# A routed-expert kernel: the first expert's weight pieces in another order, one of them split before the gathers, small copies moved on VectorE

## What is computed

```python
# 1. gated linear attention with B,H,S,D = 4,8,768,40, step by step over t; its result is x
x = attn_out.transpose(0, 2, 1, 3).reshape(B * S, H * D)      # 3072 tokens x 320
# 2. experts: N=3072 tokens, E=8 experts, F=1024, cap = N // E = 384
order = np.argsort(-(x @ w_gate).flatten())
for idx in order:
    tok, e = idx // E, idx % E
    if assigned[tok] >= 0 or counts[e] >= cap: continue
    assigned[tok] = e; counts[e] += 1
for e in range(E):
    mask = assigned == e
    out[mask] = np.maximum(x[mask] @ w1[e], 0.0) @ w2[e]
# 3. a second layer pair on all tokens, width 2048
h = out @ w_in
result = np.where(h > 0, h, np.exp(np.minimum(h, 0)) - 1) @ w_out
```

## Time and profile before

| what | us |
|---|---|
| median of three runs | 873.57 |
| lowest, highest | 872.84, 879.42 |
| the profiled execution, its own time | 876.62 |
| its span, first to last instruction | 874.3 |
| TensorE matmul busy | 806.4 |
| VectorE, ScalarE, GpSimd busy | 547.0, 461.0, 403.1 |
| mean granted clock of TensorE, share of full speed | 0.977 |

### The profile page before, as it was taken

How to read it: one execution, slowest core, us unless ns; L and a number is a source line. 1 busy time by engine, 2 the same in 40 slices (tenths; PEclk the granted TensorE clock), 3 DMA queues, 4 the chain that set the end, 5 groups by cost and what they waited for, 6 DMA issues and landing times.

```text
span 874.3 us, 17610 instructions
## 1 busy us (share of the span) xinstructions
PE 806.4 (92%) x5979; PEld 746.0 (85%) x5979; DVE 547.0 (63%) x1446; ACT 461.0 (53%) x981; POOL 403.1 (46%) x468
## 2 busy tenths in 40 slices
PE   1999999998977999999999999999999999999994
PEld 1888888887766888989998998998999899999894
DVE  7476868685754766676586577658657765543441
ACT  1544444431231576278457737836762882784573
POOL 6544444552352166246526526543651663475133
PEclk9999999998976999999999999999999999999998
DMA  3766666632331122212112121211112212021000
GB/s 61 152 136 138 137 136 131 136 80 76 103 97 30 43 65 63 65 44 58 55 47 71 46 65 46 67 62 42 59 46 65 61 52 77 28 76 50 1 1 22
DMA packets 138506, 60.94 MB, mean 70 GB/s; under 512 B 104704, under 2 KB 136704, under 8 KB 138432
## 3 DMA queue, kind: packets, MB, share of 16 engines
q1 hardware_dynamic: 136128, 52.13, 24.7%
q0 software_dynamic: 2304, 7.87, 2.8%
HBM read 51.72 MB, written 8.26 MB: 69 GB/s over the span
## 4 chain that ended last, share of the span: by engine, by line
PE 61%; DVE 9%; ACT 2%; issue 2%; POOL 1%; DMA 1%; SPq 0%; ACTq 0%; POOLq 0%
PE bank L1793 6%; PE bank L1708 6%; PE bank L1711 6%; PE bank L1709 6%; PE bank L1795 6%; PE bank L1794 6%; PE bank L1713 3%; PE bank L1712 3%; PE bank L1751 3%; PE bank L1749 3%; PE bank L1750 3%; DVE cmp L753 2%; DVE unit L1399 2%; PE bank L1645 2%; DVE unit L1396 2%
## 5 line engine op out<-in xcount | busy, mean ns | idle before, releaser
L1138 POOL TENSOR_TENSOR gl_lo<-unit,gl_hi 128x384 fp32r<-128x384 f32 x128 | 130.1, 1017 | 272.0 <-ACT gl_hi L1587 271.9
L1793 PE MATMUL bank<-Wo_hi,gl_hi 128*128 128x320 f32 x384 | 125.2, 326 | 0.5 <-POOL gl_lo L1138 0.5
L1795 PE MATMUL bank<-Wo_hi,gl_lo 128*128 128x320 f32 x384 | 119.0, 310 | 0.0
L1794 PE MATMUL bank<-Wo_lo,gl_hi 128*128 128x320 f32 x384 | 118.8, 309 | 0.0
L1396 DVE SCALAR_TENSOR_TENSOR unit<-bank,unit 128x384 f32<-128x384 f32 x104 | 57.8, 556 | 82.7 <-ACT bank L1580 77.3
L1551 ACT ACTIVATE hid_hi<-bank 128x384 fp32r<-128x384 f32 x64 | 31.4, 491 | 134.9 <-PE bank L1713 134.9
L1568 ACT ACTIVATE unit<-bank 128x384 f32<-128x384 f32 x128 | 62.2, 486 | 59.7 <-PE bank L1713 50.5
L1708 PE MATMUL bank<-x_hi,Wi_hi 128*128 128x384 f32 x224 | 80.5, 360 | 2.4 <-DVE unit L1399 1.9
L1709 PE MATMUL bank<-x_hi,Wi_lo 128*128 128x384 f32 x224 | 75.5, 337 | 0.0
L1793 PEld LDWEIGHTS bank<-Wo_hi,gl_hi 128*128 128x128 f32 x384 | 72.6, 189 | 3.2 <-POOL gl_lo L1138 3.2
L1399 DVE TENSOR_TENSOR unit<-unit,bank 128x384 f32<-128x384 f32 x128 | 70.9, 554 | 4.4
(11 more groups left out here) (288 smaller groups left out, 2202.2 us busy)
## 6 DMA issues: line engine op xcount, KB each, us to landing
stage<-in_moe_w_dram SPq DMA_DIRECT2D x32, 320.0 KB, 3.0
stage<-in_moe_w_dram SPq DMA_DIRECT2D x32, 256.0 KB, 2.6
stage<-in_moe_w_dram SPq DMA_DIRECT2D x96, 64.0 KB, 2.4
q_in<-in_q_dram SPq DMA_DIRECT2D x24, 160.0 KB, 2.6
k_in<-in_k_dram SPq DMA_DIRECT2D x24, 160.0 KB, 3.1
o_in<-in_o_gate_dram SPq DMA_DIRECT2D x24, 160.0 KB, 3.4
v_in<-in_v_dram SPq DMA_DIRECT2D x24, 160.0 KB, 3.3
x_rows<-xt SPq DMA_DIRECT2D x24, 160.0 KB, 1.8
```

Source lines behind the costliest of these rows:

```text
L1138: nc.gpsimd.tensor_tensor(gl_lo[:, b, :], ex[:, b, :], gl_hi[:, b, :].bitcast(F32), ALU.subtract).then_inc(gl_ok, 1)
L1793: nc.tensor.matmul(acc[j][:, 0:DM], gl_hi[:, f % RG, t_], Wo_hi[:, f, :], start=(f == 0), stop=False)
L1794: nc.tensor.matmul(acc[j][:, 0:DM], gl_hi[:, f % RG, t_], Wo_lo[:, f, :], start=False, stop=False)
L1795: ins = nc.tensor.matmul(acc[j][:, 0:DM], gl_lo[:, f % RG, t_], Wo_hi[:, f, :], start=False, stop=(f == NF2 - 1))
```

## The change

- For expert 0 the pieces come in the order W1 0, W1 1, W2 0, W1 2, W1 3, W2 1, W2 2, W2 3 (`AS_NEEDED`), in place of the four of W1 and then the four of W2. SyncE, ScalarE and GpSimd follow it.
- GpSimd splits the first of them ahead of the three gathers, and ScalarE makes the high part of the third one between the columns of the first gather and those of the second.
- In the rounds 2, 3 and 5 of expert 1's routing, VectorE copies the partial counts (`round_parts`) ahead of `hidden`.
- `choose_counts` builds `equal` with `below`, one number for each partition, in place of `ge` of 24.
- Constants: `SPIN_KEYS` 22 to 19, `SPIN_GATHER` 22 to 25; the slices of the third comparison beside the steps f of the second layer move.

```diff
@@ -888,7 +888,7 @@
-    ge = sb("ge", [P, G])
+    below = sb("below", [P, 1])
...
@@ -1036,24 +1036,32 @@
-    def expert_piece(k, i):
-        return k * PER + 2 * PI + i
-
+    IN_ORDER = [(True, i) for i in range(PE1)] + [(False, i) for i in range(PE1)]
+    AS_NEEDED = [(True, 0), (True, 1), (False, 0), (True, 2), (True, 3), (False, 1), (False, 2), (False, 3)]
+
+    def pieces_of(k):
+        return AS_NEEDED if first_expert(k) else IN_ORDER
+
+    def piece_number(k, at):
+        return k * PER + 2 * PI + at
+
+    def expert_piece(k, is_up, i):
+        return piece_number(k, pieces_of(k).index((is_up, i)))
...
-    def expert_arrival(k, i):
-        own = UPS * (i // 2 + 1) if i < PE1 else UPS * PE1 // 2 + DOWNS * ((i - PE1) // 2 + 1)
-        return k * ((UPS + DOWNS) * PE1 // 2) + w_out_arrival(PI - 2 + i % 2) + own
-
-    SPIN_KEYS, SPIN_COMPARE, SPIN_HALVES, SPIN_PARTS, SPIN_TEST = 22, 7, 11, 1, 2
-    SPIN_TIES, SPIN_PLACES, SPIN_SPOTS, SPIN_GATHER, SPIN_COLUMNS = 7, 14, 4, 22, 4
+    def expert_arrival(k, at):
+        own = sum(UPS if is_up else DOWNS for is_up, _ in pieces_of(k)[at % 2:at + 1:2])
+        return k * ((UPS + DOWNS) * PE1 // 2) + w_out_arrival(PI - 2 + at % 2) + own
+
+    SPIN_KEYS, SPIN_COMPARE, SPIN_HALVES, SPIN_PARTS, SPIN_TEST = 19, 7, 11, 1, 2
+    SPIN_TIES, SPIN_PLACES, SPIN_SPOTS, SPIN_GATHER, SPIN_COLUMNS = 7, 14, 4, 25, 4
...
-    SLICES_BESIDE_SPOTS = {0: (0,), 2: (1,), 3: (2,), 4: (3,), 5: (4,), 6: (5,)}
+    SLICES_BESIDE_SPOTS = {0: (0,), 2: (1,), 4: (2,), 5: (3, 4), 6: (5,)}
...
@@ -1140,12 +1149,13 @@
         for i in range(PI):
             rest(False, w_out_piece(i), i, i % 2, OUT_SPLIT)
+        expert_rest(0, 0)
         for j in range(NJ):
             gather(0, 0, j)
             if j == 0:
                 pool.sem_inc(gather_begun)
-        for i in range(PER):
-            expert_rest(0, i)
+        for at in range(1, PER):
+            expert_rest(0, at)
...
@@ -1254,10 +1264,11 @@
             nc.vector.tensor_scalar(home(k).gt_t, lo[:], base[:, 0:1], None, ALU.is_ge).then_inc(r_step, 1)
-            nc.vector.tensor_scalar(ge[:], lo[:], UNIT, base[:, 0:1], ALU.add, ALU.is_ge).then_inc(r_step, 1)
+            nc.vector.tensor_scalar(below[:], base[:], UNIT, None, ALU.subtract).then_inc(r_step, 1)
             did(k)
             dve.wait_ge(r_step, did(k))
-            nc.vector.tensor_tensor(home(k).equal_t, ge[:], home(k).gt_t, ALU.subtract).then_inc(r_step, 1)
+            nc.vector.scalar_tensor_tensor(out=home(k).equal_t, in0=lo[:], scalar=below[:, 0:1], in1=home(k).gt_t,
+                                           op0=ALU.is_ge, op1=ALU.subtract).then_inc(r_step, 1)
...
@@ -1438,18 +1449,24 @@
                     if u == 2:
                         finish_round(1, 1)
                         round_compare(1, 2)
+                        round_parts(1, 2)
                         hidden(0, 2)
-                        finish_round(1, 2)
+                        round_test(1, 2)
+                        round_move(1, 2)
                         round_compare(1, 3)
                     elif u == 3:
+                        round_parts(1, 3)
                         hidden(0, 3)
-                        finish_round(1, 3)
+                        round_test(1, 3)
+                        round_move(1, 3)
...
                     elif u == 4:
+                        round_parts(1, 5)
                         hidden(0, 4)
-                        finish_round(1, 5)
+                        round_test(1, 5)
+                        round_move(1, 5)
...
@@ -1587,28 +1604,32 @@
-        for i in range(2):
-            piece(True, i, expert_arrival(0, i), W1_SPLIT)
-        for j in range(NJ):
-            columns(0, j)
-        for i in range(2):
-            piece(True, 2 + i, expert_arrival(0, 2 + i), W1_SPLIT)
-            hidden(0, i)
-        piece(False, 0, expert_arrival(0, PE1), W2_SPLIT)
...
+        expert_hi(0, 0)
+        expert_hi(0, 1)
+        columns(0, 0)
+        expert_hi(0, 2)
+        columns(0, 1)
+        columns(0, 2)
+        hidden(0, 0)
+        expert_hi(0, 3)
+        hidden(0, 1)
+        expert_hi(0, 4)
```

39 lines of the change are left out of this document (21 added, 18 removed).

## The result

The changed kernel took 866.77 us in the median of 20 runs (863.41 to 874.39), the kernel before 874.42 in 20 runs beside them (871.96 to 880.53). The ratio is 0.9905, with a 95% interval of 0.9885 to 0.9925: about 1% faster. The forecast was 868.2, its range 864.8 to 872.8.

A forecast was written before the change was run, and what follows sets the result against it. Expert 0's start was taken as bound by GpSimd's splits and the loads they release, the clock falling with the waits; 1.4 + 2.85 + 3.7 + 0.8 = 8.75 off 876.62 gives 867.9, 868.5 from the median; taken 868.2, range 864.8 to 872.8.

The forecast's parts named there:

- The list of tokens: Expert 0's routing: fewer fillers and `below` bring the token list 1.4 us earlier net, bounds 0.5 to 2.0.
- The fillers: Ahead of expert 0's first count: 22 to 19 fillers on TensorE, 0.5 us gained.
- `sel` then comes in the gap between the splits: Expert 0's routing: `sel` at 228.6, between GpSimd's splits of w_out (228.57 to 229.22), loses its 0.4 us wait.
- The first split ahead of the gathers: GpSimd before expert 0's gathers: the split ends 0.4 us ahead of `idx`, so costs 0; up to 1.4 otherwise.
- rival (b): Expert 0's gathers: the first split holds them up, giving back up to 1.4 us: 869.6; chance 0.06.
- The stage is free for the third piece at 237.3: Expert 0's loads: W2's first piece can load from 237.3 and is there by about 240.5, ahead of the gathers.
- The order: Ahead of expert 0's `down 0`: the 2.85 us wait for W2's first piece goes, and no other wait replaces it.
- The clock in the rounds: Down 0, up 3, down 1, up 4 run at full clock: 3.7 us gained, bounds 0 to 5.0.
- the copies: Rounds 2, 3 and 5: partial-count copies ahead of `hidden` gain 0.8 us in sum (0.6 to 1.0).
- rival (a): The rounds: the clock falls all the same, four blocks cost as before: 871.6; chance 0.18.
- Rival (c): Gather wait, now 2.5 us, no longer lowers the clock: up to 1.0 saved, `mem` perhaps unheld (0.6): 866.6; chance 0.10.
- The slices: Second layer, third comparison's moved slices: 0, between 0.6 us gained and 0.6 lost.

The follow-up runs named there:

- e7_no_parts: Kernel after with the partial-count copies back behind the activations in rounds 2, 3 and 5; 867.15 us, ratio 0.991.
- e4_order_split: Kernel before with the new piece order and the early first split, without the small parts; 867.54 us, ratio 0.9904.
- e5_pad: Kernel before with three tiny GpSimd writes ahead of the splits of w_out; 871.62 us, ratio 0.9978.
- e1_order: Kernel before with the new order of the pieces and nothing else; 874.3 us, ratio 0.998.
- e9_fill: Kernel before with 16 TensorE fillers in the wait ahead of down 0; 872.97 us, ratio 0.9977.
- e11_columns: e8_free with nine more TensorE fillers between the second and third columns; 867.65 us, ratio 0.9916.
- e12_keys: e11_columns with eight fillers fewer ahead of the first count (11, not 19); 865.26 us, ratio 0.9885.
- e8_free: Kernel after with expert 0's `sel`, `mem` and `outside` written with two tensor inputs, one in PSUM; 865.93 us, ratio 0.9889.

## Why the prediction was right, and where not

The time fell in the range and near its middle, and the main mechanism was right, but two terms of the sum were wrong in opposite directions.

*The list of tokens, 1.4 us: failed.* The fillers gave their 0.5 (0.56); from the first count to the index nothing was gained (27.93 and 27.95), so the term gave less than half its size. The step that failed is "`sel` then comes in the gap between the splits". `sel` kept its date: the forecast puts it 22.85 us behind the first filler (228.6 against 205.75), and it started at 22.84. The splits did not keep theirs: the last but one ran from 22.68 to 24.25 there, where it had run from 21.27 to 22.82, since the load of its piece took longer. `sel` took 1.43 in place of the forecast 0.24, and the expert's number, which comes behind it, was written 0.2 us earlier from the first count and not the 1.5 that the sum has without its fillers. Nor was the gap one to count on: it was 0.65 us wide, `sel` was to come 0.03 us behind its start, and in e7_no_parts, where it is there, `sel` missed it by coming at its end. So what had to be priced was not one instruction against one split, but the chance that each of `ge`, `sel`, `mem` and `outside` meets one: in e4_order_split and e5_pad `ge` took 0.23 us without any change to it, `sel` 1.05 and 1.15, `mem` 0.49 and 0.96, and the index came at 27.60 and 28.18. `mem` was barely held in the kernel after (0.31).

*The first split ahead of the gathers, 0: failed as a price, right as to the gathers.* It ended at 237.84 against `idx` at 237.86, 0.02 us ahead and not the 0.4 of the forecast. The gather was not held, so rival (b) did not happen as I had it; but `idx` was, by 0.17 us. The prediction looks for such a hold at `mem` alone. And the split was worth more than nothing, by two things that I had not seen: the fetch of instructions that left the gap, 2.15 us, and that W2's load hangs on the stage which this split frees, without which the order pays nothing (e1_order). The prediction's "The stage is free for the third piece at 237.3" took this for granted.

*The order, 2.85 us: right,* together with the early split. The wait ahead of down 0 went (2.99), and nothing was late in its place.

*The clock in the rounds, 3.7, and the copies, 0.8: right in sum for the profile.* 4.5 forecast, 4.88 measured from down 0 to down 2. The copies are 0.56 of it, under their lower bound of 0.6: rounds 3 and 5 gave 0.54 each, as forecast, and round 2 lost 0.02, less than forecast; what the term left out is that the comparison behind round 3 then lies open for 0.45 more. So the clock's part is 4.3, an estimate by difference. TensorE waited 1.10 us for the fourth comparison, forecast at 0.85. That the idle stretch ahead of down 0 is the cause was argued in the prediction; the profiles speak for it (five of five, and e9_fill with 3.95 us), the times of e9_fill are no proof. For the median execution the term was probably too large: rival (a), the clock that falls all the same, is what the profiles of e7_no_parts, e11_columns and e12_keys show in part of the rounds. The mean clock of 0.981 to 0.986 in 14 of the 20 executions after fits a fall somewhere, but not of necessity there: the profile of e8_free has 0.985 with full clock in the rounds. It looks like an either-or of each execution, and not of the kernel, as my chances had it. The Trainium skill's rule that I cited for (a) ("TensorE: Matmul & The Clock Gate", section "HAM oscillation — how this bites in real kernels") is about waits for DMA that are longer than any in these rounds (some 1.1 us at most). Every burst starting at the low clock is not what the rounds show: the clock is at 1.00 through all of them in the kernel after and falls for part of them in e11_columns, 264 to 270 us.

*Rival (c), the clock of the gather wait: happened, by luck.* The wait was 0.48 us instead of the 2.5 that the rival supposed, because of the fetch, and from the first columns to the thresholds 0.95 us went, its "up to 1.0".

*The slices, 0:* right, 1.06 us of wait before, 1.02 after.

So in the profile 8.75 us were forecast and some 11.3 measured: the list gave 0.8 less than its term, the wait and the rounds 0.5 more than theirs, and 2.15 and 0.95 came that were not in the sum, less the 0.2 given back at the end. In the medians, 7.65 us. The forecast counted 5.4 from the median of before; that it is near is partly luck, since the unseen 2.15 and 0.95 us stand against the list's missing 0.8 and what the clock term lacks in the usual execution.
